# Score matmuls of two heads on separate halves of the array's rows, ahead of the first layer

## The reference

```python
batch, n_heads, seq, head_dim = (2, 8, 768, 64);  n_sink, window = (4, 128)
scores = scale * np.matmul(q, k.transpose(0, 1, 3, 2))
keep = is_sink | in_window                  # is_sink: key < n_sink; in_window: 0 <= query - key < window
scores = np.where(keep, scores, -1000000000.0)
a = np.exp(scores - max);  a = a / (sum + 1e-09)
x = np.matmul(a, v)                         # laid out as 1536 tokens x 512
h = np.maximum(x @ w_in, 0.0);   x = h * h @ w_out            # first layer, d_ff 2048
h = x @ w_in2;  g = P(h) / (Q(h) + 1e-06);  y = g @ w_out2    # second layer, d_ff 2048
```

## Time and profile before

| | |
|---|---|
| median of 3 runs | 636.86 us (636.72 to 638.67) |
| the profiled execution's own time | 636.6 us |
| its span | 634.9 us |
| PE busy | 625.2 us, 98% of the span |
| DVE, ACT, POOL busy | 449.7, 380.2, 353.8 us |
| chain that ended last | PE 83%, DVE 12%, ACT 2% |
| granted clock of PE | full in all 40 slices |

### The profile page before, as it was taken

One profiled execution on the slowest core, in us unless ns is written; L12 is line 12 of the kernel. 1 busy time (PEld: TensorE's weight loads), 2 busy tenths in 40 slices (PEclk: granted clock), 3 DMA queues, 4 the chain that ended last, 5 costly groups with the idle time before them and its releaser, 6 DMA issues.

```text
span 634.9 us, 10375 instructions
## 1 busy us (share of the span) xinstructions
PE 625.2 (98%) x3716; PEld 586.4 (92%) x3716; DVE 449.7 (71%) x705; ACT 380.2 (60%) x859; POOL 353.8 (56%) x431
## 2 busy tenths in 40 slices
PE   8999999999999999999999999999999999999997
PEld 6889999999999999999999998888999999999995
DVE  5655655354655656443567799998999989998995
ACT  4755666365444545443222576688777877778774
POOL 6899865122333334330222478777777677777773
PEclk9999999999999999999999999999999999999999
DMA  8776311052021401000444210021001110001001
GB/s 257 234 242 233 115 42 42 1 167 83 1 84 43 141 23 62 18 2 3 130 133 131 79 57 2 1 101 51 1 1 43 70 39 0 1 2 51 1 0 56
DMA packets 28972, 43.50 MB, mean 69 GB/s; under 512 B 4080, under 2 KB 19440, under 8 KB 28400
## 3 DMA queue, kind: packets, MB, share of 16 engines
q1 hardware_dynamic: 28912, 42.74, 20.7%
HBM read 36.44 MB, written 6.29 MB: 67 GB/s over the span
## 4 chain that ended last, share of the span: by engine, by line
PE 83%; DVE 12%; ACT 2%; POOL 1%; issue 1%; DMA 0%; DVEq 0%; ACTq 0%; POOLq 0%; SPq 0%
PE h_ps L1502 24%; PE y_ps L1514 20%; PE y_ps L1817 16%; PE s_ps L1502 8%; PE o_ps L1502 4%; DVE s_ps L1191 4%; PE o_ps L1629 3%; PE s_ps L1555 2%; DVE h_ps L1191 2%; PE s_ps L1577 2%; DVE p_buf L1194 2%; DVE p_buf L1185 1%; PE s_ps L1551 1%; DVE o_ps L1191 1%; PE y_ps L1551 1%
## 5 line engine op out<-in xcount | busy, mean ns | idle before, releaser
L1502 PE MATMUL h_ps<-xT,weights 128*128 128x384 f32 x960 | 190.1, 339 | 0.4 <-DVE sq L1201 0.3
L1502 PEld LDWEIGHTS h_ps<-xT,weights 128*128 128x128 f32 x960 | 167.3, 188 | 3.8 <-issue 2.5
L1514 PE MATMUL y_ps<-hid,weights 128*128 128x384 f32 x768 | 149.8, 338 | 0.0
L1817 PE MATMUL y_ps<-weights,hid 128*128 128x512 f32 x576 | 142.6, 393 | 1.3 <-POOL hid L765 0.8
L1514 PEld LDWEIGHTS y_ps<-hid,weights 128*128 128x128 f32 x768 | 132.9, 188 | 0.7 <-issue 0.7
L1817 PEld LDWEIGHTS y_ps<-weights,hid 128*128 128x128 f32 x576 | 106.8, 188 | 22.2 <-POOL hid L765 2.3
L845 ACT ACTIVATE sq<-sq 128x384 f32<-128x384 f32 x64 | 33.4, 522 | 103.1 <-DVE sq L1201 103.0
L765 POOL TENSOR_TENSOR hid<-p_buf,hid 128x384 fp32r<-128x384 f32 x63 | 65.7, 1043 | 42.9 <-ACT hid L1071 42.5
L1160 DVE TENSOR_TENSOR hid<-sq,hid 128x384 fp32r<-128x384 f32 x64 | 47.0, 734 | 59.7 <-ACT hid L803 59.7
L1191 DVE RECIPROCAL s_ps<-q_buf 128x384 f32<-128x384 f32 x32 | 82.0, 2561 | 3.3
L756 POOL TENSOR_TENSOR q_buf<-h_abs,q_buf 128x384 f32<-128x384 f32 x64 | 65.7, 1027 | 29.0 <-ACT q_buf L821 26.7
(11 more groups left out here) (147 smaller groups left out, 886.2 us busy)
## 6 DMA issues: line engine op xcount, KB each, us to landing
weights_raw<-in_w_pack SPq DMA_DIRECT2D x32, 512.0 KB, 4.3
bk_raw<-in_k_pack SPq DMA_DIRECT2D x24, 256.0 KB, 3.9
q_pair<-in_q_pack SPq DMA_DIRECT2D x21, 256.0 KB, 3.5
bv<-in_v_pack SPq DMA_DIRECT2D x24, 128.0 KB, 2.4
y_scratch<-xT SPq DMA_DIRECT2D x2, 1536.0 KB, 6.2
xT<-y_scratch SPq DMA_DIRECT2D x2, 1536.0 KB, 6.6
out_y<-out_stage SPq DMA_DIRECT2D x3, 768.0 KB, 3.6
inv_cols<-in_q_pack SPq DMA_DIRECT2D x3, 256.0 KB, 4.4
```

The costliest lines, as they stand in the source:

```text
L1502: ins = nc.tensor.matmul(bank, weights[:, i, wp, W_IN, t * P:(t + 1) * P], x, start=(t == 0 and n == 0), stop=(t == KC - 1 and n == 2))
L1514: ins = nc.tensor.matmul(y_ps[:, m, 0:NT], weights[:, i, wp, W_OUT, m * P:(m + 1) * P], hid[:, i % 2, gp, :], start=(i == 0 and n == 0), s ...
L1817: ins = nc.tensor.matmul(y_bank(turn, t), hid2[:, i % RING, gp, t * P:(t + 1) * P], weights[:, i, wp, W_OUT, :], start=(i == 0 and n == 0) ...
```

## The change

The score matmuls of groups 0 to 7 use 64 rows of the array: even heads rows 0 to 63, odd heads rows 64 to 127. Their queries come from a new input, `q_first`, which holds the even head of a pair in the upper and the odd head in the lower 64 partitions, so that a load is 128 by 256 instead of 128 by 512 numbers. The loop of slots on PE, DVE and ACT handles two units a turn: both scores stand next to each other, then both transposes, then both weighings, of units `s - 4` and `s - 3`. `score(u)` now waits until DVE has read both units of the pair before.

```diff
-            return [qt for qt in range(QT) if (slots_before(qt) if qt + 1 < QT else LEAD - 1) == s]
+            return [qt for qt in range(QT) if (slots_before(qt) if qt + 1 < QT else LEAD - 2) == s]
...
-                sp.dma_start(queries(k), q_pack[k]).then_inc(q_loaded[q_slot(k)], 16)
+                to, of = (queries(k)[:, 0:2 * P], q_first[k]) if k < EARLY else (queries(k), q_pack[k])
+                sp.dma_start(to, of).then_inc(q_loaded[q_slot(k)], 16)
...
-                def slot(s):
-                    if s >= 2 and s % 2:
-                        pT_part(s - 2)
+                def slots(s):
                     exp(s)
-                    if with_sinks(s):
+                    exp(s + 1)
+                    if with_sinks(s + 1):
                         pack_sinks(s // GROUP)
+                    if s >= 2:
+                        pT_part(s - 1)
...
-                def slot(s):
+                def slots(s):
                     scores(s)
-                    if s >= 2 and s % 2 == 0:
+                    scores(s + 1)
+                    if s >= 2:
                         pT_part(s - 2)
...
                 if 2 <= u < LEAD:
-                    pe.wait_ge(u_negs, u - 1)
+                    pe.wait_ge(u_negs, u // 2 * 2)
...
-                    ins = nc.tensor.matmul(score_bank(u)[:, cols], queries(k)[:, at], bk_raw[:, m, cols],
+                    rows, two = slice(D * (m % 2), D * (m % 2) + D), slice(m % GROUP // 2 * P, m % GROUP // 2 * P + P)
+                    ins = nc.tensor.matmul(score_bank(u)[:, cols], queries(k)[rows, two], bk_raw[rows, m, cols],
                                            start=True, stop=True)
...
-                def slot(s):
+                def slots(s):
                     if s >= 2:
                         score(s)
+                        score(s + 1)
                         turn_p(s - 2)
-                    if 3 <= s < UNITS + 3:
+                        turn_p(s - 1)
+                    if GROUP <= s < UNITS + GROUP:
+                        weigh(s - 4)
                         weigh(s - 3)
...
-                for s in range(LEAD):
-                    slot(s)
+                for s in range(0, LEAD, 2):
+                    slots(s)
...
+    q_first = q_pack[0:8].reshape(8, dim, 2, 2, P).transpose(0, 3, 1, 2, 4).reshape(8, 2 * dim, 2 * P)
     q_pack = np.concatenate([q_pack, q_pack], axis=1)
-    q_pack[0:8, dim:, :] = 0.0
```

More of the change, by code:

```diff
@@ L25, with build @@
 LATE_W = 3
-def build(nc, q_cols, k_cols, v_rows, k_pack, q_pack, ks_pack, v_pack, vs_pack, consts_in, w_pack1, w_pack2, out):
+def build(nc, q_cols, k_cols, v_rows, k_pack, q_pack, q_first, ks_pack, v_pack, vs_pack, consts_in, w_pack1, w_pack2, out):
     B, H, D, S = q_cols.shape
@@ L1869 @@
              np.ascontiguousarray(moe2_b).reshape(-1).view(np.int32)]
-    given = dict(q_cols=q_cols, k_cols=k_cols, v_rows=v_rows, k_pack=k_pack, q_pack=q_pack, ks_pack=ks_pack, v_pack=v_pack,
+    given = dict(q_cols=q_cols, k_cols=k_cols, v_rows=v_rows, k_pack=k_pack, q_pack=q_pack, q_first=q_first, ks_pack=ks_pack, v_pack=v_pack,
                  vs_pack=vs_pack, consts=np.concatenate(words), w_pack1=by_tile(moe_w_in, moe_w_out),
```

## The result

| | before | changed |
|---|---|---|
| median of 11 runs each | 636.12 us (635.67 to 638.67) | 640.59 us (639.18 to 652.34) |
| ratio | | 1.0078, 95% interval 1.0056 to 1.0099 |
| the profiled execution's own time | 636.6 us | 647.93 us |
| its span | 634.9 us | 646.1 us |
| first layer's first matmul | 39.50 us | 51.05 us |

A forecast was written before the change was run, and what follows sets the result against it. PE was taken to bound the kernel, busy 98% of the span. Score pairs 0.4, fewer copy waits 0.3 and hand-overs 0 gave 0.7 us off 636.6: 635.9 us, range 634.1 to 637.9.

The forecast's parts named there:

- slower rivals: Score pairs with a 0.45 us toll, 638.8 us, or without any overlap, 639 us; together 14%.
- Side by side, three steps of four: Score pairs of units 0 to 31: partly overlapping matmuls make a 288-column pair cost 0.81 us instead of 1.08, before toll.
- Going in and out: Switching between half-row score pairs and whole-array work around them: a toll of 0.21 us for each pair.
- Two units a turn: PE's waits for copies at the start: 0.3 us of 0.8 us goes as PE alternates half as often.
- The hand-overs: Ends of tiles ahead of the first layer: at tile 0 a 0.4 or 0.5 us wait replaces about 0.46; nothing gained overall.
- A late load: Rival: query loads of groups 6 and 7 make PE wait up to 0.5 us; 636.4 us, chance counted within the forecast's 66%.
- From unit 32 on: After the early units: POOL has unit 32's queries ready 2.1 us before, so a 0.7 us gain passes to the end.
- the toll that turns the sum negative: Switching cost per score pair from which the change would lose time: put at 0.27 us.
- a change without overlap: Rival: row halves do not run at once in score pairs; 3.2 us slower, 639 us, within a shared 14%.

The follow-up runs named there:

- order-alone run: The kernel before with loops of two units a turn on PE, DVE and ACT, scores kept at full depth; 636.6 us, ratio 1.0005.
- half rows from unit 16: The changed kernel with the scores of units 0 to 15 at full depth again; 635.87 us, ratio 0.9989.
- half rows from unit 8: The changed kernel with the scores of units 0 to 7 at full depth again, run twice; 635.55 us and 635.89 us.
- half rows alone: The kernel before, one unit a slot, with only the score operands changed to 64 rows; 673.6 us, ratio 1.059.

## Why the prediction was wrong

**The step that failed is one that the text does not have: the level of PE's clock.** The earlier trace rows were read as what a matmul of that shape costs, and every term of the sum is a difference of such rows. They hold only at the upper level. The page said full speed in every slice, and I asked neither what had raised it at 5 us nor whether the change took that away. None of the rivals has it either. The slower rivals ended near 639 us, but by a toll at the upper level. The measured 640.59 is not theirs: that run has some 14 us at 1.2 GHz by its recorded clock, and in the two profiled runs the low level held until 38 or 47 us. There a turn of two units takes 3.90 us, against 2.30 for two slots before.

**Side by side, three steps of four: wrong, too dear.** I let PE start the four matmuls of a pair in order, so that the pair would cost 0.81 us. They start in twos (39.06 with 39.07, 39.41 with 39.41), and the pair costs 0.69. The second rule that the prediction weighed, the Trainium skill's ("TensorE: Matmul & The Clock Gate", Part 3: Packing small matmuls), fits these rows: two tiles take the time of one. What the prediction also lacks is that matmuls on half rows follow each other more slowly than at full depth, 0.34 us here from one start to the next against 0.27.

**Going in and out: right in kind and near in size.** Against the same order at full depth, the transposes are 0.06 us longer (22.26 to 22.75, against 22.93 to 23.36 in the order-alone run) and the weighings 0.09 (20.64 to 21.57, against 23.36 to 24.20), together 0.15 where I took 0.21. The 0.29 of a lone score has the same two parts and 0.14 inside the score, which a pair pays once for two. So a pair costs 0.84 where I said 1.02, and a turn without a stall is 2.11 us (0.69, 0.49 and 0.93) where two slots took 2.30: 0.19 saved, not 0.06. The Trainium skill's drain at a change of mode ("TensorEngine Tiling (Array Packing)", Tiling Modes) agrees in sign with both places.

**Two units a turn, 0.3 us: not there.** The order alone gave 636.6 against 636.32, with an interval on both sides of 1 and half a per mille above it at the middle. In its profile the waits for copies are indeed gone (0.8 us before, none there), but new ones take their place: 0.46 us for a query load at 8.63, and pair 30, 31 starts 0.66 us after `tile_out` (36.49 to 37.15) where 0.44 passed before.

**The hand-overs: partly.** Before unit 16 PE waited for DVE as forecast, but 0.20 us (19.35) and not 0.4. In that version PE scores unit 16 at 19.35, before at 19.93, and starts the first layer at 38.53, before at 39.50. Between the two only 0.39 us is gained, where seven turns of 0.19 and a last pair 0.29 shorter would give 1.6. Two things take the rest. One weighing has moved behind unit 16: the turn of units 16 and 17 weighs units 12 and 13, slot 16 weighed 13 alone, so that 12 weighings follow there and 11 before, some 0.4 us. The others are stalls that I had at nothing. Pair 20, 21 starts at 23.87 where the weighings before it would be through at 23.68: 0.19. Pair 30, 31 starts 0.83 us after `tile_out` (35.45 to 36.28) where 0.44 passed before (35.54 to 35.98); some 0.1 of these 0.39 is the price of going in, which the 0.19 a turn contains already, and 0.22 stands as a wait for DVE's copy. The second unit's transposes come 0.09 late at 20.39 and 0.17 late at 30.27. These stalls make 0.75; the last 0.1 I can't place.

**A late load: it can come.** The prediction gave it up to 0.5 us, at groups 6 and 7. In the profile of half rows from unit 16, PE waits 0.63 us for the query load of group 4 ahead of unit 16 (at 19.94).

**From unit 32 on: right.** 11.55 us late at the first layer is 11.3 at the end, and 0.97 early is 1.05 in that profiled run (635.55 against 636.6). POOL had the slack.

The level once held up, the kernel with 12 pairs on half rows comes to 635.55 and 635.89 us, which is the forecast of 635.9; but two of my errors (a pair too dear, stalls too few) cancel there, so that is no credit to the working. At the median this version is ahead of the kernel before by 0.6 us in one series and 0.4 in the other, but the second interval takes in 1.

Two small sums of the prediction are off as well. With 0.7 us gained over 15 pairs the toll that turns the sum negative is 0.26, not 0.27, and a change without overlap, 3.2 us slower, would end near 639.8 us, not 639. Nothing hangs on either.

Open: when the level rises, and why it differs from run to run of one kernel. The changed kernel has low stretches from some 10 to 37 us long with the same instructions. With the first pairs at full depth the rise came by 5.6 us (before), at about 7 us (order alone) or 11.6 us (half rows from unit 8). Nothing in the rows ahead of the rise tells the runs apart. What in a half-row score holds the level down is not shown either, only that it goes with the depth.

## What to carry to other kernels

Before you price a change at a kernel's start, read which level PE's matmuls run at there, and ask which of them it removes: full-depth matmuls that multiply by zero may be what brings the level up, as here. Check the level by the spacing of one shape early and late, not by the clock row alone. Where a tiling of the rows pays, let it begin once the level is up, and use it in pairs: a lone score on half rows cost 0.29 us more here than at full depth.

## What the runs showed that I had not expected

- Half-row matmuls can hold PE at its lower level through nearly unbroken work (from 5 to 76 us with the half rows alone), and in one profile the level fell from the upper in the midst of them (at 9.2 us).
- The row of granted clock can read full where the spacing of matmuls is that of the lower level: until 38.3 us in the changed kernel, and until 76 us with the half rows alone. In the second profile of the changed kernel, where a fall was recorded, it reads 0.50.
- Two row halves run wholly at once, each product's two matmuls included: 0.69 us for two heads, 0.68 for one.
- Added idle products at full depth made the changed kernel faster, 637.4 us at the median against 640.6 and 648.0.
